# Changing the expert in four steps over two iterations, with two row buffers, earlier gathers and a second first-layer bank

## The chip, the cores and the metric

The kernel runs on one core of a Trainium2 chip. The core has TensorE (PE, matmuls into PSUM banks; PEld is its weight load), VectorE (DVE), ScalarE (ACT), GpSimd (POOL) and SyncE (SP), each with its own instruction stream; they wait for one another through semaphores. The metric is the device time of one execution in microseconds; lower is better.

## What is computed

Three stages follow one another. `_attn_ref` is attention with four sink keys and a window of 128 over 4 batches, 8 heads, 768 positions. `_moe_ref` is a dense layer, 512 to 2048 and back, with `h - tanh(h)` between. The third stage sends each of the 3072 tokens to one of eight experts:

```python
logits = x @ w_gate + modality_bias[modality_id]
e_idx = np.argmax(logits, axis=1)
...
for e in range(E):
    mask = e_idx == e
    if not mask.any():
        continue
    h = np.maximum(x[mask] @ w1[e], 0.0)
    out[mask] = gate_w[mask, None] * (h @ w2[e])
```

`w1[e]` is 512 x 1024 and `w2[e]` is 1024 x 512. In the profiled data the trace shows the weights of two experts loaded, so the expert changes once.

## The kernel before

**Front.** The dense layer works on eight chunks of 384 tokens. Chunk m has 16 column blocks f. `mlp_in` computes the first layer of block f into the bank `h_ps` (12 matmuls); ACT takes the tanh (L718), DVE subtracts it (L727, "the gate of f"), ACT and DVE split the result into a high and a low 16-bit half (`g_hi` L737, `g_lo` L747), and `mlp_out` multiplies them with `w_out` (9 matmuls). PE runs `mlp_in` of f+1 ahead of `mlp_out` of f. Since there is one bank, `mlp_in` of f+2 waits until the gate of f+1 has read it. In the last chunk the first expert is prepared between: DVE and ACT look for the largest weights (`look_over`), and split the eight weight pieces into `ew_hi` and `ew_lo` (L1474, L1478). Then the routing of the last chunk is computed.

**Expert stage.** Tokens are sorted by expert in a table `slots`, and worked off in blocks of 128, numbered j from 0 to 24. For a block, POOL loads its part of the table (`load_slots`, tile `slot_g`) and gathers its rows of `x2` (`gather`, tile `xg`); DVE finds the scale and ACT applies it (`scale_x`, L1723 to L1730); PE transposes (`transpose_x`, L1743, into `x_out`); ACT and DVE split (`xg_hi` L1749, `xg_lo` L1752). `hidden_products` is 96 small matmuls (L1766) in two halves c of four column groups; `relu` splits each half (`hid_hi` L1780, `hid_lo` L1783). `output_products` is 24 matmuls of 512 columns (L1817). `load_slots_again` fetches the gate weights (`slot_y`, L1791), DVE makes `y_scale` of them (`output_scale`, L1805), ACT scales the output (`y`, L1833), POOL scatters it (L1838).

Blocks 0 to 2 are "early" blocks of the first expert, and their code is written out. Block 3 is the joining block: `output_products` of block 2 alone, then `transpose_x` of 3, then `hidden_products` of 3 alone. From j = 4 a loop runs: in iteration j PE interleaves `hidden_products` of j with `output_products` of j-1, one large matmul with four small ones, and transposes j+1 after the 15th large one. At its start PE waits for `y_set` of at least j-1, which is `output_scale` of the iteration before, the last thing that DVE does in an iteration. The order on ACT and DVE is what `iteration` writes.

**Tables.** DVE computes the plan on one partition: `plan`, `plan_blocks` (raises `planned`), and `plan_late` (raises `planned_late`; every engine waits for it ahead of the loop, and SP ahead of loading the next expert). The loop's conditions, whether a block begins an expert, are read from this plan by `read` (L1609) and tested by a branch.

**Change of expert.** `load_turn` loads the eight pieces of the next expert as soon as the present one has been split. `look_ahead` runs in the iteration after the first block of an expert. `next_turn` runs in the last iteration of the old expert (13 begins the new one, so j = 12): new scales, then, when all hidden products of block 12 are done, the four pieces of `w1`; in the next iteration, when the outputs of block 12 are done, the four pieces of `w2`.

Of the kernel before, what the change touches and what calls it, by code (L numbers as in the profile page):

```python
# [25 lines left out]
P = 128  # L26
# [26 lines left out]
PIECES = 8  # L53
NEG = -1.0e9
# [63 lines left out]
def front(nc, dram, shared, attention):  # L118

    with ExitStack() as ctx:  # L120
# [59 lines left out]
        h_ps, x_out = h_bank[:, 0:CT], x_bank[:, 0:CT]  # L180
# [509 lines left out]
        def mlp_in(E, eng, m, f, between=None):  # L690
# [4 lines left out]
            if E == "pe":  # L695
# [4 lines left out]
                need(eng, q["g_done"], n)  # L700
                i = 0
                for x, r in ((1, xt_hi), (0, xt_lo), (0, xt_hi)):
                    if i == 2 * KD and between:
                        between()
                    for k in range(KD):
                        mm = eng.matmul(h_ps, w16[0][:, f, x * DM + k * P:x * DM + (k + 1) * P], r[:, par, k, :],  # L706
                                        start=(i == 0), stop=(i == 3 * KD - 1))
                        i += 1
                mm.then_inc(q["h_done"], 1)
            if E == "act":  # L710
# [7 lines left out]
                eng.activation(g_raw[:, f % 2, :], h_ps, ACT.Tanh, scale=batch_scale[:, b, 0:1]).then_inc(q["tanh_done"], 1)  # L718

        def mlp_gate(E, eng, m, f):  # L720
# [184 lines left out]
        def prepare_expert(E, eng, k):  # L905
# [9 lines left out]
            if k in (15, 17, 19, 21):  # L915
                shared.split(E, eng, 0, (k - 15, k - 14))
# [76 lines left out]
        def join(E, eng):  # L993
# [9 lines left out]
            if E == "dve":  # L1003
# [332 lines left out]
class Shared:  # L1336
# [33 lines left out]
    def over_attention(self, sb):  # L1370
# [73 lines left out]
    def set_scales(self, E, eng, s, bank=None):  # L1444
# [9 lines left out]
        need(eng, self.w_hi, PIECES * s)  # L1454
# [12 lines left out]
    def split(self, E, eng, s, pieces):  # L1467

        for i in pieces:
            scale = self.w_scale[:, 0:1] if i < KD else self.w_scale[:, 1:2]  # L1470
            hi, lo = self.hi[:, i, :], self.lo[:, i, :]
            if E == "act":
                eng.wait_ge(self.scaled, s + 1)
                eng.activation(hi, self.raw[i][:], ACT.Copy, scale=scale).then_inc(self.w_hi, 1)  # L1474
            if E == "dve":
                eng.wait_ge(self.scaled, s + 1)
                eng.wait_ge(self.w_hi, PIECES * s + i + 1)
                eng.scalar_tensor_tensor(lo, self.raw[i][:], scale, hi, ALU.mult, ALU.subtract).then_inc(self.w_lo, 1)  # L1478
# [74 lines left out]
    def plan_late(self, eng):  # L1553
# [11 lines left out]
        step(tt(metaf[:, 2, :], vec["first"][:], b[:], ALU.mult))  # L1565
# [9 lines left out]
def expert_stage(sb, sem, dram, shared, xt_ps, hid_ps, y_ps):  # L1575
# [10 lines left out]
    slot_g = sb("slot_g", [P, 2], I32)  # L1586
# [44 lines left out]
    def next_turn(E, eng, j):  # L1631
# [61 lines left out]
    def load_slots(E, eng, j):  # L1693

        if E == "pool":
# [341 lines left out]
```

## Time and profile before

| | |
|---|---|
| median of 3 runs | 1139.35 us (1139.07 to 1141.08) |
| profiled execution | 1141.86 us, span 1140.2 us |
| PE busy | 1017.1 us, 89% of the span |
| DVE, ACT, POOL busy | 729.6, 618.5, 397.3 us |
| mean granted clock of TensorE | 0.972 of full speed |

The span is from the first to the last instruction; what lies around it is 1.7 us. PE is the engine with the most work, so idle time of PE, and time in which its clock is half, is what an edit can take away or add.

### The profile page before, as it was taken

The page shows a single profiled execution, that of the slowest core. Times are in us where ns is not written, and L with a number is a line of the kernel's source. Part 1 is how long each engine was busy: PE and PEld are TensorE (multiplying, and loading weights), DVE is VectorE, ACT ScalarE, POOL GpSimd, SP SyncE. Part 2 cuts the span into 40 slices and gives each one's busy share as a digit, 9 for nine tenths or more (in the row PEclk, how much of TensorE's full clock was granted, in tenths as well). Part 3 has the DMA queues.
Part 4 walks back from the last instruction along what each step waited for, and adds up shares of the span by engine and source line. Part 5 has one row for each costly group of instructions (what it writes and reads, how often), then busy time and mean ns, then how long its engine had stood idle before and what let it go on. Part 6 is the DMA issues. An engine that isn't in the chain of part 4 may idle for free.

```text
span 1140.2 us, 24342 instructions
## 1 busy us (share of the span) xinstructions
PE 1017.1 (89%) x7840; PEld 664.2 (58%) x7840; DVE 729.6 (64%) x2388; ACT 618.5 (54%) x1421; POOL 397.3 (35%) x457
## 2 busy tenths in 40 slices
PE   1657888999999999999999999998896999789997
PEld 0534555565665665566566566654664677567774
DVE  6787978677977867887867876547563333443331
ACT  2675877575766766667666667445322222332221
POOL 3786876222345312325412321110122222122222
PEclk9976999999999999999999999999998999889999
DMA  9832111231212322311231130050023111001111
GB/s 284 282 97 53 34 34 34 75 109 34 61 37 63 62 90 58 69 35 34 38 90 34 34 61 2 1 203 2 29 79 136 43 46 56 28 23 52 46 46 45
DMA packets 24427, 75.14 MB, mean 66 GB/s; under 512 B 9680, under 2 KB 9808, under 8 KB 22800
## 3 DMA queue, kind: packets, MB, share of 16 engines
q1 hardware_dynamic: 15440, 60.58, 19.9%
q0 software_dynamic: 5728, 13.43, 3.8%
q8 instruction: 44, 0.72, 0.3%
q14 instruction: 47, 0.39, 0.1%
q10 hardware_dynamic: 3168, 0.02, 0.1%
HBM read 60.16 MB, written 14.12 MB: 65 GB/s over the span
## 4 chain that ended last, share of the span: by engine, by line
PE 67%; DVE 15%; ACT 6%; issue 6%; POOL 2%; DMA 2%; DVEq 0%; ACTq 0%; SPq 0%; POOLq 0%
PE h_ps L706 16%; PE acc L762 14%; PE pt_ps L1766 11%; PE h_ps L1817 6%; PE acc L1817 5%; PE x_out L665 4%; PE s_ps L542 2%; PE pt_ps L611 2%; DVE g_raw L727 2%; DVE qk_top L385 2%; DVE qk_exp L394 1%; PE s_ps L811 1%; DVE ew_lo L1478 1%; DVE g_lo L747 1%; ACT probs L557 1%
## 5 line engine op out<-in xcount | busy, mean ns | idle before, releaser
L762 PE MATMUL acc<-w_out_all,g_hi 128*128 128x512 f16 x768 | 228.3, 379 | 0.0
L706 PE MATMUL h_ps<-xt_hi,w_in_all 128*128 128x384 f16 x1024 | 211.1, 329 | 16.9 <-DVE g_raw L727 16.8
L762 PE MATMUL acc<-w_out_all,g_lo 128*128 128x512 f16 x384 | 145.4, 379 | 2.5 <-POOL w_out_all L350 1.2
L594 ACT ACTIVATE pt_hi<-pt_ps 128x256 f16<-128x256 f32 (+2 forms) x224 | 83.6, 380 | 110.0 <-PE pt_ps L611 106.0
L706 PEld LDWEIGHTS h_ps<-xt_hi,w_in_all 128*128 128x128 f16 x1024 | 97.6, 99 | 78.2 <-DVE g_raw L727 16.3
L98 POOL TENSOR_TENSOR tick<-tick 1x1 f32<-1x1 f32 x83 | 15.3, 184 | 313.0 <-ACT y L1833 97.8
L747 DVE SCALAR_TENSOR_TENSOR g_lo<-g_raw,batch_scale,g_hi 128x384 f16<-128x384 f32 x128 | 95.2, 743 | 33.1 <-ACT g_hi L737 30.7
L762 PEld LDWEIGHTS acc<-w_out_all,g_hi 128*128 128x128 f16 x768 | 75.0, 98 | 69.2
L598 DVE TENSOR_TENSOR pt_lo<-pt_ps,pt_hi 128x256 f16<-128x256 f32 (+2 forms) x224 | 94.3, 423 | 29.9 <-ACT pt_hi L594 28.2
L718 ACT ACTIVATE g_raw<-h_ps,batch_scale 128x384 f32<-128x384 f32 x128 | 74.3, 580 | 71.8 <-PE h_ps L706 70.5
L432 POOL TENSOR_TENSOR q_stack<-qk_raw,q_stack 64x768 f16<-64x768 f32 x31 | 50.8, 1639 | 165.5 <-ACT q_stack L428 165.5
L706 PE MATMUL h_ps<-xt_lo,w_in_all 128*128 128x384 f16 x512 | 106.1, 331 | 0.0
L575 ACT ACTIVATE normed<-probs,row_sum 128x260 f32<-128x260 f32 (+1 forms) x192 | 92.9, 484 | 21.1 <-DVE row_sum L570 20.9
L727 DVE SCALAR_TENSOR_TENSOR g_raw<-h_ps,batch_scale,g_raw 128x384 f32<-128x384 f32 x128 | 78.4, 612 | 37.9 <-ACT g_raw L718 36.5
L737 ACT ACTIVATE g_hi<-g_raw,batch_scale 128x384 f16<-128x384 f32 x128 | 78.0, 609 | 45.2 <-DVE g_raw L727 44.7
L1783 DVE SCALAR_TENSOR_TENSOR hid_lo<-pt_ps,hid_hi 128x512 f16<-128x512 f32 x50 | 34.6, 691 | 96.5 <-ACT hid_hi L1780 91.9
L557 ACT ACTIVATE probs<-probs,neg_max 128x260 f32<-128x260 f32 (+1 forms) x192 | 92.8, 483 | 5.8 <-DVE neg_max L552 5.7
L432 POOL TENSOR_TENSOR kl_stack<-qk_raw,kh_stack 128x1048 f16<-128x1048 f32 (+1 forms) x31 | 60.2, 1941 | 99.1 <-ACT kh_stack L428 98.4
L611 PE MATMUL pt_ps<-ident,normed 128*128 128x128 f32 x352 | 74.0, 286 | 22.7 <-ACT normed L575 22.6
L552 DVE CUSTOM_DVE_ANT_0 probs<-s_ps,mask 128x260 f32<-128x260 f32 (+1 forms) x180 | 73.1, 406 | 24.1 <-issue 22.9
L1766 PE MATMUL pt_ps<-xg_lo,ew_hi 128*128 128x128 f16 x800 | 79.0, 222 | 1.5 <-DVE xg_lo L1752 1.4
L409 POOL TENSOR_SCALAR qk_raw<-qk_raw,qk_scale 128x768 f32<-128x768 f32 (+2 forms) x62 | 61.0, 996 | 52.3 <-DVE qk_scale L400 52.3
(293 smaller groups left out, 2237.3 us busy)
## 6 DMA issues: line engine op xcount, KB each, us to landing
qk_raw<-in_qk SPq DMA_DIRECT2D x64, 454.0 KB, 6.1
raw<-in_w SPq DMA_DIRECT2D x16, 512.0 KB, 7.7
v_raw<-in_v SPq DMA_DIRECT2D x4, 1536.0 KB, 9.7
x_tokens<-x SPq DMA_DIRECT2D x24, 256.0 KB, 5.3
w_in_all<-in_w_in SPq DMA_DIRECT2D x4, 1024.0 KB, 13.2
w_out_all<-in_w_out SPq DMA_DIRECT2D x4, 1024.0 KB, 12.3
x_tokens<-g_raw SPq DMA_DIRECT2D x1, 1024.0 KB, 14.0
slots<-payload,dest POOLq DMA_INDIRECT x24
```

The lines of the kernel that those rows point to most:

```text
L432: eng.tensor_tensor(lo, raw[half], hi[half], ALU.subtract).then_inc(q["conv_lo"], 1)
L557: eng.activation(probs[:, r, cols], probs[:, r, cols], ACT.Exp, bias=neg_max[:, r:r + 1], scale=-1.0, accum_out=row_sum[:, r:r + 1]).then_ ...
L575: eng.activation(normed[:, u % 6, cols], probs[:, r, cols], ACT.Copy, scale=row_sum[:, r:r + 1])\
L594: eng.activation(pt_hi[:, at, :], out, ACT.Copy).then_inc(q["pt_hi_done"], 1)
L598: eng.tensor_tensor(pt_lo[:, at, :], out, pt_hi[:, at, :], ALU.subtract).then_inc(q["pt_lo_done"], 1)
L611: mm = eng.transpose(out[:, b, :], normed[:, u % 6, b * KB:b * KB + P], ident[:])
L706: mm = eng.matmul(h_ps, w16[0][:, f, x * DM + k * P:x * DM + (k + 1) * P], r[:, par, k, :], start=(i == 0), stop=(i == 3 * KD - 1))
L727: eng.scalar_tensor_tensor(g, h_ps, batch_scale[:, b, 0:1], g, ALU.mult, ALU.subtract).then_inc(q["g_done"], 1)
L747: eng.scalar_tensor_tensor(g_lo[f % 2][:], g, batch_scale[:, b, 1:2], g_hi[f % 2][:], ALU.mult, ALU.subtract)\
L762: mm = eng.matmul(acc[t][:, :], l[f % 2][:, t * P:(t + 1) * P], w16[1][:, f, x * DM:(x + 1) * DM], start=(f == 0 and i == 0), stop=(f == N ...
L1766: mm = eng.matmul(hid_ps[c][:, (f - 4 * c) * P:(f - 4 * c + 1) * P], w[:, k, f * P:(f + 1) * P], x[p][:, k * P:(k + 1) * P], start=(i == 0 ...
L1817: mm = eng.matmul(y_ps[bank][:, :], l[:, f * P:(f + 1) * P], rhs, start=(f == 0 and i == 0), stop=(f == KF - 1 and i == 2))
```

## The change

1. **Four steps.** The weights of the next expert are split in quarters: `w1` first half of the columns in iteration J-1 (J is the first block of the new expert) after half c = 0 of J-1 is done; `w1` second half at the head of iteration J; `w2` first two pieces in iteration J after `y_half`; `w2` last two at the head of iteration J+1. The head is ahead of `relu` of j-1. New scales are made by DVE in iteration J-1 ahead of `relu` of j. `look_ahead` moves from the iteration after the expert's first block to two iterations ahead of J (iteration J-2), and stands ahead of `relu` of j. `load_slots_again` moves ahead of the transposed rows. In an iteration without any step, ACT and DVE now test more conditions.
2. **Two row buffers.** `xg` and `slot_g` have two halves, so `gather` of j+2 waits for the transposes of j, not of j+1. The slots and rows of block 4 are fetched directly after those of block 3, ahead of the early scatters.
3. **Order.** `transpose_x` in an iteration comes after the 18th large matmul, not the 15th. In the joining block it stands inside the products, and the early `scale_x` goes ahead of the output of block 1. `plan_late`, with five more steps, moves from ahead of the joining block to behind it. SP loads the next expert after three gathers.
4. **Two banks.** In the last chunk `mlp_in` writes odd f into `pt_bank[1]`, and waits for one gate less.

```diff
+        def h_of(m, f):
+            return (pt_bank[1] if m == NC - 1 and f % 2 else h_bank)[:, 0:CT]
...
-                need(eng, q["g_done"], n)
+                need(eng, q["g_done"], n - 1 if m == NC - 1 and f else n)
...
                 stage_e.relu(E, eng, 2, 0)
-                shared.plan_late(eng)
...
-                stage_e.load_slots(E, eng, EARLY)
-                stage_e.gather(E, eng, EARLY)
+                stage_e.load_slots(E, eng, EARLY, EARLY % 2)
+                stage_e.gather(E, eng, EARLY, EARLY % 2)
+                eng.wait_ge(shared.planned, 1)
+                stage_e.load_slots(E, eng, EARLY + 1, 1 - EARLY % 2)
+                stage_e.gather(E, eng, EARLY + 1, 1 - EARLY % 2)
...
-        step(tt(metaf[:, 2, :], vec["first"][:], b[:], ALU.mult))
+        first, now, sel, short = vec["first"], metaf[:, 1, :], vec["n"], vec["t"]
+        w = MB - KD
+        step(ts(metaf[:, 2, :], b[:], 0.0, None, ALU.mult))
+        step(tt(sel[:, 0:w], now[:, 0:w], now[:, 2:w + 2], ALU.is_equal))
+        step(tt(sel[:, 0:w], sel[:, 0:w], first[:, 3:w + 3], ALU.mult))
+        step(tt(short[:, 0:w], first[:, 0:w], first[:, 2:w + 2], ALU.mult))
+        step(tt(sel[:, 0:w], sel[:, 0:w], short[:, 0:w], ALU.add))
+        step(tt(metaf[:, 2, 0:w], sel[:, 0:w], b[:, 0:w], ALU.mult))
...
+    def next_turn_begins(E, eng, j):
 
         if E in ("act", "dve"):
             s = read(eng, 4, j + 1, NE)
             with eng.If(s > 0):
-                shared.set_scales(E, eng, s)
-                eng.wait_ge(q["hid_mm"], 2 * j + 2)
-                shared.split(E, eng, s, range(KD))
+                eng.wait_ge(q["hid_mm"], 2 * j + 1)
+                shared.split_w1(E, eng, s, 0)
             s = read(eng, 4, j, NE)
             with eng.If(s > 0):
-                eng.wait_ge(q["y_mm"], j)
-                shared.split(E, eng, s, range(KD, PIECES))
+                eng.wait_ge(q["y_half"], j)
+                shared.split_w2(E, eng, s, 0)
+
+    def next_turn_ends(E, eng, j):
+
+        if E in ("act", "dve"):
+            s = read(eng, 4, j, NE)
+            with eng.If(s > 0):
+                eng.wait_ge(q["hid_mm"], 2 * j)
+                shared.split_w1(E, eng, s, 1)
+            s = read(eng, 4, j - 1, NE)
+            with eng.If(s > 0):
+                eng.wait_ge(q["y_mm"], j - 1)
+                shared.split_w2(E, eng, s, 1)
...
         if E == "dve":
+            next_turn_ends(E, eng, j)
             relu(E, eng, j - 1, 1)
             output_part(E, eng, j - 1, 1 - p, turn_of(eng, j - 1))
             scale_x(E, eng, j + 1, 1 - p)
+            look_ahead(E, eng, j)
+            next_scales(E, eng, j)
             relu(E, eng, j, 0)
+            next_turn_begins(E, eng, j)
             transpose_x(E, eng, j + 1, 1 - p)
-            look_ahead(E, eng, j)
-            next_turn(E, eng, j)
             output_scale(E, eng, j - 1, j - EARLY)
```

On POOL, where the early blocks end, the rows of before are these (tick is the one-element operation that carries the waits):

```order
L1702 DMA slot_g<-slots 128x2
L98 TENSOR_TENSOR tick<-tick 1x1 [waits e_slot_in]
L1710 DMA xg<-x_tokens,slot_g 128x512
L98 TENSOR_TENSOR tick<-tick 1x1 [waits e_y_out]
L1838 DMA out<-y,slot_e 3072x512
L98 TENSOR_TENSOR tick<-tick 1x1 [waits e_carried_3,e_y_out]
L1838 DMA out<-y,slot_e 3072x512
```

And these at the same place of the change:

```order
L1747 DMA slot_g<-slots 128x2
L99 TENSOR_TENSOR tick<-tick 1x1 [waits e_slot_in]
L1755 DMA xg<-x_tokens,slot_g 128x512
L1636 TENSOR_LOAD meta [waits planned]
L1636 ISA x2
L99 TENSOR_TENSOR tick<-tick 1x1 [waits e_carried_1]
L1747 ISA
L1747 DMA slot_g<-slots 128x2
L99 TENSOR_TENSOR tick<-tick 1x1 [waits e_carried_2,e_slot_in]
L1755 DMA xg<-x_tokens,slot_g 128x512
L99 TENSOR_TENSOR tick<-tick 1x1 [waits e_y_out]
L1884 DMA out<-y,slot_e 3072x512
```

The second fetch has moved ahead of the scatter of block 0. On DVE, at the end of the joining block, before:

```order
L1752 TENSOR_TENSOR xg_lo<-x_out,xg_hi 128x512 [waits e_xt_hi]
L1609 TENSOR_LOAD meta [waits planned]
L1609 ISA x2
L1965 UNCONDITIONAL_BRANCH [waits planned_late]
```

And in the change, where the plan's steps are left out in the middle:

```order
L1798 TENSOR_TENSOR xg_lo<-x_out,xg_hi 128x512 [waits e_xt_hi]
L1582 TENSOR_SCALAR vec_b<-metaf 1x44
L1583 TENSOR_SCALAR vec_t<-vec_b,pt_turn_end 1x44 [waits plan_late_step]
...
L1598 COPY metaf<-pt_turn_end 1x1 [waits plan_late_step]
L1599 CAST meta_late<-metaf 1x132 [waits plan_late_step]
L1636 TENSOR_LOAD meta [waits planned]
L1636 ISA x2
L2015 UNCONDITIONAL_BRANCH [waits planned_late]
```

The late plan, 18 rows in all, now stands between the last split of the joining block and the entry of the loop.

## Rows read from the trace of the kernel before

**Rows 1.** Waits of PE, 822 us to the end: total us, times, longest:
```profile
PE h_ps L1817 <- DVE y_scale L1805: 11.6, 2, 6.7
PE x_out L1743 <- ACT xg L1730: 6.9, 1, 6.9
PE acc L1817 <- DVE y_scale L1805: 6.1, 1, 6.1
```

**Rows 2.** Waits of PE, 740 to 822 us (the last chunk):
```profile
PE h_ps L706 <- DVE g_raw L727: 3.6, 3, 1.7
```

**Rows 3.** Timeline, last chunk, ACT: start, us, engine, line, operation [idle before]:
```profile
809.62 0.58 ACT L718 ACTIVATE g_raw<-h_ps,batch_scale 128x384 f32<-128x384 f32 x1 [0.34 <-PE h_ps L706]
```

**Rows 4.** Windows of iterations 4, 5, 10 to 14: length, busy PE, PEld, DVE, ACT, POOL, clock, DMA, GB/s:
```profile
868.70:886.38 17.68, 12.80 (x124) 8.97 (x125) 9.13 (x17) 6.81 (x13) 2.96 (x5) 0.89 0.11 31
886.38:898.86 12.48, 12.44 (x124) 9.04 (x124) 3.69 (x10) 3.07 (x6) 3.17 (x6) 0.89 0.26 55
942.82:953.80 10.98, 10.98 (x128) 8.20 (x125) 3.69 (x10) 3.09 (x6) 3.16 (x6) 1.00 0.15 47
953.80:964.83 11.03, 11.03 (x128) 8.20 (x125) 3.69 (x10) 3.14 (x6) 3.16 (x6) 1.00 0.16 48
964.83:982.75 17.92, 11.18 (x127) 8.19 (x125) 10.05 (x22) 7.46 (x10) 3.16 (x6) 0.96 0.10 30
982.75:1002.61 19.86, 13.71 (x125) 9.83 (x125) 8.48 (x14) 7.36 (x10) 3.16 (x6) 0.84 0.08 27
1002.61:1016.44 13.83, 13.83 (x124) 10.00 (x124) 3.70 (x10) 3.06 (x6) 3.16 (x6) 0.79 0.09 21
```

**Rows 5.** Timelines of the joining block, POOL, ACT, DVE, PE:
```profile
837.72 0.58 POOL L1702 DMA_DIRECT2D slot_g<-slots  x1 [0.45 <-issue]
...
841.80 1.03 POOL L1838 DMA_INDIRECT out<-y,slot_e  x1 [0.16 <-POOL tick L98]
...
847.09 0.69 ACT L1833 ACTIVATE y<-acc,ye_scale 128x512 f32<-128x512 f32 x1 [4.45 <-PE acc L1817]
...
843.28 0.16 DVE L1562 TENSOR_SCALAR vec_b<-metaf 1x44 f32<-1x44 f32 x1
...
846.71 0.22 DVE L1572 CAST meta_late<-metaf 1x132 int32<-1x132 f32 x1
...
868.70 0.60 PE L1817 MATMUL acc<-ew_hi,hid_lo 128*128 128x512 f16 x1 [0.82 <-issue]
```

**Rows 6.** DMA issues, 925 to 1100 us: queue, kind, count, KB, us to landing:
```profile
slot_y<-slots ACTq DMA_DIRECT2D x14, 1.0 KB, 1.7
out<-y,slot_y POOLq DMA_INDIRECT x14, 2.8
```

**Rows 7.** DMA issues, 848 to 866 us (while the next expert loads):
```profile
slot_g<-slots POOLq DMA_DIRECT2D x2, 1.0 KB, 4.0
```

**Rows 8.** Timelines of iteration 9, which begins at 931.83 us, ACT and DVE:
```profile
931.82 0.69 ACT L1833 ACTIVATE y<-acc,y_scale 128x512 f32<-128x512 f32 x1 [3.27 <-PE acc L1817]
...
933.03 0.69 DVE L1783 SCALAR_TENSOR_TENSOR hid_lo<-pt_ps,hid_hi 128x512 f16<-128x512 f32 x1 [1.30 <-ACT hid_hi L1780]
...
935.45 0.15 DVE L1727 TENSOR_SCALAR x_undo<-x_exp 128x1 int32<-128x1 int32 x1
...
939.59 0.69 DVE L1752 TENSOR_TENSOR xg_lo<-x_out,xg_hi 128x512 f16<-128x512 f32 x1 [0.93 <-ACT xg_hi L1749]
942.45 0.16 DVE L1805 TENSOR_TENSOR y_scale<-slot_y,y_part 128x1 f32<-128x1 f32 x1 [2.17 <-DMA slot_y<-slots]
```

**Rows 9.** The chain in order of time, a read and branch on DVE, and the next:
```profile
972.70 0.31 DVEq L1609
...
973.64 0.31 DVEq L1609
```

**Rows 10.** Timelines of iterations 4 and 12, DVE: the work of the change of expert:
```profile
879.09 4.60 DVE L1415 TENSOR_REDUCE tops<-raw 128x1 f32<-128x1024 f32 x4 [0.24 <-issue]
...
977.67 4.87 DVE L1478 SCALAR_TENSOR_TENSOR ew_lo<-raw,ew_scale,ew_hi 128x1024 f16<-128x1024 f32 x4 [1.22 <-ACT ew_hi L1474]
```

More of the change, by code:

```diff
@@ L717, in mlp_in @@
                 need(eng, q["g_hi_done"], n - 1)
[L718 removed]
+                eng.activation(g_raw[:, f % 2, :], h_of(m, f), ACT.Tanh, scale=batch_scale[:, b, 0:1]).then_inc(q["tanh_done"], 1)
         def mlp_gate(E, eng, m, f):
@@ L915, in prepare_expert @@
             if k in (15, 17, 19, 21):
-                shared.split(E, eng, 0, (k - 15, k - 14))
+                shared.split_first(E, eng, (k - 15, k - 14))
             if k == 23:
@@ L1453, in set_scales @@
             source = bank[:, 0:2 * P].rearrange("p (i n) -> p i n", i=2)
-        need(eng, self.w_hi, PIECES * s)
+        need(eng, self.w_hi, PARTS * s)
         step = chain(eng, self.scale_step, 7 * s)
@@ L1465, in set_scales, with split_part, split_first, split_w1 @@
         eng.tensor_tensor(at, self.both[:, 0:1], self.both[:, 1:2], ALU.mult).then_inc(self.scaled, 1)
-    def split(self, E, eng, s, pieces):
-        for i in pieces:
[L1470 to L1478, printed above, removed]
+    def split_part(self, E, eng, s, n, i, cols, counted=1):
+        scale = self.w_scale[:, 0:1] if i < KD else self.w_scale[:, 1:2]
+        raw, hi, lo = self.raw[i][:, cols], self.hi[:, i, cols], self.lo[:, i, cols]
+        if E == "act":
+            eng.wait_ge(self.scaled, s + 1)
+            eng.activation(hi, raw, ACT.Copy, scale=scale).then_inc(self.w_hi, counted)
+        if E == "dve":
+            eng.wait_ge(self.scaled, s + 1)
+            eng.wait_ge(self.w_hi, PARTS * s + n + 1)
+            eng.scalar_tensor_tensor(lo, raw, scale, hi, ALU.mult, ALU.subtract).then_inc(self.w_lo, counted)
+    def split_first(self, E, eng, pieces):
+        for i in pieces:
+            self.split_part(E, eng, 0, KD + i, i, slice(0, FE), counted=KD + 1 if i == 0 else 1)
+    def split_w1(self, E, eng, s, half):
+        for i in range(KD):
+            self.split_part(E, eng, s, KD * half + i, i, slice(half * FE // 2, (half + 1) * FE // 2))
+    def split_w2(self, E, eng, s, pair):
+        for i in (2 * pair, 2 * pair + 1):
+            self.split_part(E, eng, s, 2 * KD + i, KD + i, slice(0, FE))
     def plan_iotas(self, eng):
@@ L1629, in look_ahead, with next_scales @@
                 shared.sum_rows(E, eng, s)
-    def next_turn(E, eng, j):
+    def next_scales(E, eng, j):
+        if E == "dve":
+            s = read(eng, 4, j + 1, NE)
+            with eng.If(s > 0):
+                shared.set_scales(E, eng, s)
+    def next_turn_begins(E, eng, j):
         if E in ("act", "dve"):
@@ L1699, in load_slots, with gather @@
                 row = read(eng, 0, j, NE * N - P)
-            need(eng, q["gathered"], 16 * (j - EARLY))
+            need(eng, q["gathered"], 16 * (j - EARLY - 1))
             carry_waits(eng, tick, 7, q["carried_1"], j - EARLY)
-            eng.dma_start(slot_g[:], dram["slots"][bass.ds(row, P), :]).then_inc(q["slot_in"], 16)
-    def gather(E, eng, j):
+            eng.dma_start(slot_g[:, p, :], dram["slots"][bass.ds(row, P), :]).then_inc(q["slot_in"], 16)
+    def gather(E, eng, j, p):
         if E == "pool":
             eng.wait_ge(q["slot_in"], 16 * (j - EARLY + 1))
-            if not (isinstance(j, int) and j == EARLY):
-                eng.wait_ge(q["xt_done"], j)
+            if not (isinstance(j, int) and j < EARLY + 2):
+                eng.wait_ge(q["xt_done"], j - 1)
             carry_waits(eng, tick, 2, q["carried_2"], j - EARLY)
-            eng.indirect_dma_start(out=xg[:], out_offset=None, in_=dram["x2"],
-                                   in_offset=bass.IndirectOffsetOnAxis(ap=slot_g[:, 0:1], axis=0)).then_inc(q["gathered"], 16)
+            eng.indirect_dma_start(out=xg[:, p, :], out_offset=None, in_=dram["x2"],
+                                   in_offset=bass.IndirectOffsetOnAxis(ap=slot_g[:, p, 0:1], axis=0)).then_inc(q["gathered"], 16)
     def scale_x(E, eng, j, p):
         n = j - EARLY
+        x = xg[:, p, :]
         if E == "dve":
@@ L1871, in iteration @@
             scale_x(E, eng, j + 1, 1 - p)
+            look_ahead(E, eng, j)
+            next_scales(E, eng, j)
             relu(E, eng, j, 0)
+            next_turn_begins(E, eng, j)
             transpose_x(E, eng, j + 1, 1 - p)
-            look_ahead(E, eng, j)
-            next_turn(E, eng, j)
             output_scale(E, eng, j - 1, j - EARLY)
         if E == "pool":
-            load_slots(E, eng, j + 2)
-            gather(E, eng, j + 2)
+            load_slots(E, eng, j + 2, p)
+            gather(E, eng, j + 2, p)
             output(E, eng, j - 1, 1 - p)
```

62 lines of the change are left out of this document (33 added, 29 removed).

## The prediction

> **What bounds the kernel now.** I read the waits of PE first. From 822 us to the end PE waited 11.6 and 6.1 us for `y_scale` and 6.9 us for the scaled rows `xg` [rows 1]: 24.6 us, all at the joining block, in iteration 4 and at the change of expert. In the last chunk it waited 3.6 us for the gate [rows 2]. Then the windows that run from one start of an iteration to the next [rows 4]. An undisturbed iteration takes 10.98 us with PE busy throughout, so such iterations can't get shorter. Iteration 4 took 17.68, 5 took 12.48, 11 took 11.03, 12 to 14 took 17.92, 19.86 and 13.83. The clock column shows the second cost: a wait of PE is followed by a stretch at the lower of its two levels (mean 0.89 in iteration 5, 0.79 in iteration 14, where PE never idled and still lost 2.85 us). So there are 24.6 us of waits and some 6 us of clock to be had (17.68, 12.48, 17.92, 19.86 and 13.83 hold 26.9 us above five times 10.98, and the joining block the rest); the rest of PE's work is not touched.
>
> **Last chunk.** The second bank lets `mlp_in` run before the gate of the block ahead, but `mlp_out` still needs that block's `g_lo`, and the gates come one behind the other on DVE, which is also splitting the first expert. DVE has the same list as before, so PE's 3.6 us [rows 2] mostly move to the wait for `g_lo`. What is won is what ACT then waits less for its last tanh: it sat idle 0.34 us before it [rows 3]. I take 0.4; the bounds are 0 and 3.6.
>
> **Joining block.** All times here are on the clock of the old trace.
> - POOL: the scatter of block 0 was issued at 841.80, one slot load (837.72) and one gather behind [rows 5]. A second pair, 4.08 us by those two rows, plus a read of some 0.5 us, is now ahead of it: 846.4. It lands 2.8 us later [rows 6]: 849.2.
> - ACT's output of block 1 needs that landing, and stood at 847.09 [rows 5]: now 849.2. Behind it on ACT is `relu` of block 2, half 1; from output to the end of `hid_lo` takes 1.9 us (931.82 to 933.72, [rows 8]): 851.1.
> - PE starts the lone output products at 847.1, does 12 of 24 and the transposes of block 3 (12 x 0.22 + 0.44: these and 96 x 0.055 make up 10.98 [rows 4]): 850.2. It waits 0.9 us, does the other 12 (853.8), and hidden products with the transposes of 4 (5.3 + 0.44): 859.6. The wait of 6.9 us for `xg` [rows 1] is gone, because the rows of block 4 were fetched seven us earlier.
> - But `plan_late` is now behind DVE's last split of block 4. PE transposes block 4 at 857.8; the split ends some 1.9 us later, 859.7. The plan took 3.65 us (843.28 to 846.93 [rows 5]), and five more steps of 0.22 us make 4.75: 864.4. Every engine waits for it before the loop. The way into the loop was 0.82 us [rows 5], of which the read is now done before; I take 0.5. PE's loop begins at 864.9, less 0.4 from the chunk: 864.5 instead of 868.70. **Won: 4.2**, and there is a new wait of PE of 5.3 us for the plan. Bounds: 2.5 (the scatter lands 1.7 us later) and 9 (no wait for the plan).
>
> **Iteration 4.** `look_ahead` leaves it: four reductions of 4.60 us on DVE [rows 10], behind which `y_scale` stood. The 17.68 us fall to 10.98 plus the slow clock after the new wait, 1.5 us as in iteration 5 (12.48), so 12.5. But SP now loads the 4 MB of the next expert during it, since it waits for the plan and three gathers. The slot load that `y_scale` needs takes 1.7 us alone [rows 6]; POOL's small load under such traffic took a median 4.0 [rows 7]. I add 0.6: 13.1. **Won: 4.6** (bounds 3 and 6). Iteration 5 then has no wait ahead of it, 12.48 to 10.98: **won 1.5**.
>
> **Ordinary iterations.** Each has more reads with a branch: ACT 6 for 4, DVE 7 for 4. One costs 0.94 us on DVE [rows 9]; on ACT, where no two stand bare, I take 0.85. They count only where the engine is waited for. With T the start on PE: ACT's output at T, two tests, `hid_hi` at T+1.75, `hid_lo` at T+2.35 (before T+1.2); from there to `x_undo` 2.42 us (933.03 to 935.45 [rows 8]): T+4.8; ACT's scaling and one test, `hid_hi` of c = 0 at T+5.8; slot load and two tests, T+8.7; PE's transposes after the 18th product are ready at T+8.5; `xg_hi` 8.7, `xg_lo` 9.35, `y_scale` 10.1. PE needs it at about T+10.7. Before, it was ready at T+10.6 [rows 8], since three tests stood between `xg_lo` and it (939.59 to 942.45). So 0.6 us is spare: cost nothing, with 0.4 us once, in iteration 20, where the outer loop turns. Bounds: 0 and 1.5 us for each of 16 iterations.
>
> The Trainium skill (Runtime: NRT & Kernel Launch, Instruction fetch mechanics) says that a taken branch to a target outside the pages already held has to wait for a fetch. The rows show 0.94 us for a test whose branch is taken over its body, with nothing larger, so the sum goes by the row; by the rule the longer bodies could make some tests dearer, which is the slower rival below.
>
> **Change of expert, iterations 11 to 14.** Each is worked out as a chain on ACT and DVE.
> - 11: `look_ahead` begins on DVE at T+5.75 and takes 4.6; with the row sums and the test for new scales, `hid_lo` of c = 0 starts at 11.65; two tests, `xg_lo` 13.6, `y_scale` 14.3. **14.6 us.**
> - 12: the outer loop turns (0.8 on ACT); new scales, 1.9 us, are done at 9.4; `hid_lo` 9.5; four half-size splits (half of 4.87 [rows 10]) from 10.5 to 13.0; `xg_lo`, `y_scale` 13.7. **14.0.**
> - 13: four half-size splits at the head, so `hid_lo` of half 1 at 4.05 to 4.7, just ahead of PE's need at 5.25; `x_undo` 6.45, two tests, `hid_lo` 8.4; two tests; two full splits behind ACT's, 11.4 to 13.8; `xg_lo`, `y_scale` 14.5. **14.8.**
> - 14: two full splits at the head, `hid_lo` 5.2 to 5.9 (PE waits 0.65); the rest as in an ordinary iteration, 1.5 to 2 us later: **13.2.**
>
> Sum 56.6 against 11.03 + 17.92 + 19.86 + 13.83 = 62.64 [rows 4]: **won 6.0**. PE idles between 2 and 4 us ahead of 12, 13 and 14. Whether its clock falls there matters little, as DVE sets the end of these iterations. Bounds: 0 won (each chain 1.5 us longer) and 18.7 (all four at 10.98).
>
> **Sum.** 4.2 + 4.6 + 1.5 + 6.0 - 0.4 = 15.9 us. The profiled execution took 1141.86 us (span 1140.2 and 1.7 around it) and would take 1126.0; it stands 2.5 us above the median of the runs. From the median: 1139.35 - 15.9 = **1123.5**.
>
> **The rivals.**
> - *The steps hide almost wholly.* For it: the sequencers run ahead of queued work whose waits are met, so the tests may cost less than 0.9 us. Against it: most instructions here do wait. Iterations 11 to 14 at 12 us each win 14.6 instead of 6.0, and with the small terms at their better bounds: about 1112.
> - *The late plan and the late load take the gain.* The plan behind the joining block is at its dear bound, and the 4 MB delay the slots and rows of blocks 6 and 7, so that iteration 4 wins 3; with 4 from the change of expert: 2.5 + 3 + 1.5 + 4 - 0.4 = 10.6, so 1129.
> - *Only the join is gained; the four steps cost what they save.* Iterations 11 to 14 stay at 62.6: 1129.5. For it: DVE's list is as long as before.
> - *Slower: the tests become the bound.* Each of the 16 ordinary iterations (5 to 10 and 15 to 24) ends when ACT and DVE are through their tests. With 0.6 us spare, six tests in series would have to cost 0.27 us more apiece to add 1.0 us to an iteration; 15.9 / 16 = 1.0 us each is where it decides, and at 1.3 us each the time is 1144. Against it: the price of a test is read from a row.
> - *No change:* nothing in the trace speaks for it; the waits for `xg` and `look_ahead` are surely gone.
>
> **How the numbers follow.** Forecast 0.55 (its own range 1118 to 1127), steps hidden 0.15, late load 0.12, steps cost what they save 0.10, slower 0.06, within 0.2% 0.02 (2.3 us, about what a measurement of this kernel can tell from no change). The range from 1114 to 1131 leaves out part of the first rival and the last two, about 2 in 10. Faster 0.92, same 0.02, slower 0.06.
>
> **What would show it.** PE waits some 5 us before the first matmul of the loop, released by the plan; no wait for `xg`. The next expert's load begins near 866 us, after the loop's start. Iteration 4 takes about 13 us, ordinary ones 10.98. Iterations 11 to 14 take 13 to 15 us each, with `y_scale` as PE's releaser. If ordinary iterations exceed 11.2 us, the price of the tests was wrong; if 11 to 14 are near 11, the chains; if the loop begins before 862, the plan was not in the way.

## The result and the profile after

The changed kernel takes 1127.51 us (median of 4 runs, 1126.34 to 1129.42), beside 1140.21 us for the kernel before (1139.07 to 1143.89). The ratio is 0.9885 (95% interval 0.9857 to 0.9912): 1.15% faster. The forecast of 1123.5 us was 4.0 us too low. The stated range of 1114 to 1131 held; the forecast's own narrower one, 1118 to 1127, was missed by 0.5 us. The profiled execution took 1126.34 us, span 1124.7 us, 15.5 us less than before.

The waits of PE from 822 us to the end, beside [rows 1]:

```profile
PE acc L1863 <- DVE y_scale L1851: 6.6, 2, 3.9
PE acc L1863 <- issue: 5.8, 1, 5.8
PE h_ps L1863 <- DVE y_scale L1851: 4.6, 3, 3.0
PE h_ps L1863 <- DVE hid_lo L1829: 2.2, 2, 1.6
PE h_ps L1863 <- issue: 1.7, 1, 1.7
```

The wait for `xg` is gone, and a wait "issue" of 5.8 us is new: it is the wait ahead of the loop. What PE waits for `y_scale` fell from 17.7 to 11.2 us. The two waits for `hid_lo` are 0.64 us, which was there before too, and 1.61 us in the joining block. In the last chunk, beside [rows 2], the three waits for the gate are gone, and there are these:

```profile
PE s_ps L866 <- DVE payload L851: 3.2, 1, 3.2
PE acc L766 <- DVE g_lo L751: 1.3, 1, 1.3
```

The iterations 4, 5, 10, 11, 12, 13, 14 and 15, one line each, in windows with the columns of [rows 4]:

```profile
863.65:878.52 14.87, 13.64 (x125) 9.77 (x125) 3.69 (x10) 2.55 (x5) 1.95 (x4) 0.83 0.82 299
878.52:889.50 10.98, 10.98 (x124) 8.17 (x125) 3.60 (x10) 3.17 (x6) 3.15 (x6) 1.00 0.16 54
933.46:944.44 10.98, 10.98 (x128) 8.18 (x126) 3.60 (x10) 3.20 (x6) 3.16 (x6) 1.00 0.15 48
944.44:958.30 13.86, 11.16 (x128) 8.19 (x126) 8.42 (x16) 7.27 (x14) 3.15 (x6) 1.00 0.14 38
958.30:972.41 14.11, 11.15 (x124) 8.18 (x125) 7.79 (x22) 5.64 (x10) 3.15 (x6) 1.00 0.24 47
972.41:987.60 15.19, 11.33 (x125) 8.15 (x125) 8.73 (x16) 7.71 (x12) 3.37 (x6) 1.00 0.11 35
987.60:1000.80 13.20, 12.80 (x124) 9.21 (x125) 5.90 (x12) 5.26 (x8) 3.27 (x6) 0.87 0.09 22
1000.80:1011.78 10.98, 10.97 (x124) 8.19 (x125) 3.60 (x10) 3.18 (x6) 3.15 (x6) 1.00 0.15 48
```

Iterations 11 to 14 last 56.36 us together against 62.64, with the DVE work of the change (8.42, 7.79, 8.73, 5.90 us busy) spread over four of them where it lay in two and in iteration 4. Iteration 4 lasts 14.87 us against 17.68.

**Where the 15.5 us came from.** In the profiled executions of all kernels here the first 810 us differ by up to 3.9 us, also between kernels that are alike there. So I count from one instruction near the end of the last chunk: the last group of PE's transposes of `xe` there, which begins with its 1.0 us wait for `xg_lo`. Before and after it reads:

```profile
812.97 0.63 PE L1743 MATMUL x_out<-ident,xe 128*128 128x128 f32 x4 [1.01 <-DVE xg_lo L1752]
```

```profile
810.35 0.63 PE L1789 MATMUL x_out<-ident,xe 128*128 128x128 f32 x4 [1.01 <-DVE xg_lo L1798]
```

Up to there the changed kernel is 2.62 us ahead: 3.15 us of that were gained before the last chunk began, and the chunk itself is 0.53 us longer (each from the DVE row that writes `x` at the end of one chunk to the same row of the next, 740.63 to 812.96 against 743.78 to 815.58). From the mark to the loop's first matmul it was 55.73 us and is 53.30 (won 2.43). Then come iteration 4 (2.81), 5 to 10 (1.50) and 11 to 14 (6.28); the rest lost 0.14. Sum 2.62 + 2.43 + 2.81 + 1.50 + 6.28 - 0.14 = 15.5. Without the 3.15 us ahead of the last chunk, where the two kernels are alike, 12.35 us are left: the change's own share. Below, "the rest from the mark" is the span less the start of this instruction: 327.23 us before, 314.35 after.

### The profile page after: what moved, and what is told of

Same layout as the page of the kernel before. It is cut to its first block, busy times and chain, and to the rows that moved or that the text cites. A ratio compares the mean times of both kernels' runs of the same rounds, so it can differ in the third digit from the quotient of the medians.

```text
span 1124.7 us, 24805 instructions
## 1 busy us (share of the span) xinstructions
PE 1010.4 (90%) x7840; PEld 660.9 (59%) x7840; DVE 728.9 (65%) x2397; ACT 620.1 (55%) x1425; POOL 396.8 (35%) x457
## 4 chain that ended last, share of the span: by engine, by line
PE 63%; DVE 16%; issue 7%; ACT 6%; POOL 3%; DMA 2%; ACTq 1%; DVEq 1%; POOLq 0%; SPq 0%
PE h_ps L710 16%; PE acc L766 15%; PE pt_ps L1812 9%; PE x_out L669 5%; PE h_ps L1863 4%; PE acc L1863 4%; PE s_ps L546 2%; PE pt_ps L615 2%; DVE qk_top L389 2%; DVE qk_exp L398 1%; PE s_ps L815 1%; DVE g_raw L731 1%; DVE ew_lo L1483 1%; DVE pt_lo L602 1%; ACT probs L561 1%
## 5 line engine op out<-in xcount | busy, mean ns | idle before, releaser
L710 PE MATMUL h_ps<-xt_hi,w_in_all 128*128 128x384 f16 x960 | 197.1, 328 | 13.2 <-DVE g_raw L731 13.2
L710 PEld LDWEIGHTS h_ps<-xt_hi,w_in_all 128*128 128x128 f16 x960 | 91.6, 98 | 67.5 <-issue 10.1
L722 ACT ACTIVATE g_raw<-h_ps,batch_scale 128x384 f32<-128x384 f32 x120 | 69.5, 579 | 64.7 <-PE h_ps L710 63.1
L710 PE MATMUL h_ps<-xt_lo,w_in_all 128*128 128x384 f16 x480 | 99.0, 329 | 0.0
L731 DVE SCALAR_TENSOR_TENSOR g_raw<-h_ps,batch_scale,g_raw 128x384 f32<-128x384 f32 x120 | 73.5, 612 | 31.8 <-ACT g_raw L722 30.7
L1812 PE MATMUL pt_ps<-xg_hi,ew_lo 128*128 128x128 f16 x800 | 78.3, 221 | 0.0
```

Source lines behind the costliest of these rows:

```text
L710: mm = eng.matmul(h_of(m, f), w16[0][:, f, x * DM + k * P:x * DM + (k + 1) * P], r[:, par, k, :], start=(i == 0), stop=(i == 3 * KD - 1))
L731: eng.scalar_tensor_tensor(g, h_of(m, f), batch_scale[:, b, 0:1], g, ALU.mult, ALU.subtract).then_inc(q["g_done"], 1)
L1812: mm = eng.matmul(hid_ps[c][:, (f - 4 * c) * P:(f - 4 * c + 1) * P], w[:, k, f * P:(f + 1) * P], x[p][:, k * P:(k + 1) * P], start=(i == 0 ...
```

## The experiments

Each edit is against the changed kernel unless it says otherwise.

**The change once more** (`after_again`), no edit.

> The change itself once more. If the 1.6 us wait of PE in the joining block and the slot load of 3.2 us ahead of it were of that one execution, they are absent here, the loop begins about 49 us after the last chunk's last matmul, and the span is some 1.6 us shorter than 1124.7; if they belong to the change, both are there again.

1125.56 us (1125.42 to 1127.74), ratio 0.9883 (0.985 to 0.9917). The rest from the mark (812.29, span 1123.8) is 311.51 us, 2.84 less than in the first profile. The loop begins at 863.79, 51.50 after the mark and not 53.30, and the 1.6 us wait for `hid_lo` isn't there. POOL's timeline shows why, first of the first execution, then of this one (a `tick` that waits marks the landing of the slots):

```profile
835.38 0.58 POOL L1747 DMA_DIRECT2D slot_g<-slots  x1 [0.45 <-issue]
838.61 0.18 POOL L99 TENSOR_TENSOR tick<-tick 1x1 f32<-1x1 f32 x1 [2.64 <-DMA slot_g<-slots]
...
844.42 1.03 POOL L1884 DMA_INDIRECT out<-y,slot_e  x1 [0.16 <-POOL tick L99]
```

```profile
836.54 0.58 POOL L1747 DMA_DIRECT2D slot_g<-slots  x1 [0.39 <-issue]
838.64 0.18 POOL L99 TENSOR_TENSOR tick<-tick 1x1 f32<-1x1 f32 x1 [1.52 <-DMA slot_g<-slots]
```

The same 1 KB load took 3.2 us once and 2.1 us here. It had also been issued later in the first execution, 25.03 us after the mark against 24.25, because the writing of `slots` ahead of it had landed 0.8 us later. Both shifted everything behind them on POOL, the scatter of block 0 among it, by 2.1 us; the loop's start moved by 1.8.

Iteration 4 was 13.77 us here and 14.87 there, and that is mostly the clock. The wait ahead of the loop was the same, 5.8 us, but behind it six matmuls of 512 columns took 0.60 to 0.64 us in the first execution and four here, so PE was busy 13.64 us against 12.83. The window here, beside the first of those above:

```profile
863.79:877.56 13.77, 12.83 (x124) 9.30 (x125) 3.69 (x10) 2.55 (x5) 1.95 (x4) 0.87 0.88 321
```

The load of `slot_y` was issued 0.8 us later for it; from issue to `y_scale` it took 5.77 us against 5.48. So of the 2.84 us between two executions of one kernel, some 1.8 are two small DMAs ahead of the loop, 0.8 are the clock behind one and the same wait, and 0.3 a third DMA. Why these differ isn't shown.

**One bank** (`one_bank`):

```diff
-            return (pt_bank[1] if m == NC - 1 and f % 2 else h_bank)[:, 0:CT]
+            return h_bank[:, 0:CT]
...
-                need(eng, q["g_done"], n - 1 if m == NC - 1 and f else n)
+                need(eng, q["g_done"], n)
```

> The changed kernel with the second first-layer bank taken out again; all else is kept. Theory A (the second bank only gathers three short waits of PE into one of 3.2 us at the ranking matmul, behind which the clock falls): the last chunk, from the store of the chunk before to the end of its own products, gets 0.5 to 1.4 us shorter than with two banks, the three waits of 1.7, 1.4 and 1.0 us come back, and no matmul of the second layer takes 0.6 us. Time 1126 to 1127.5. Rival B (the second bank wins what PE waited for the gate): the chunk gets 1 to 3 us longer, time 1129 to 1131.

**The second bank alone, in the kernel before** (`bank_only`, the same lines put in there):

> The kernel before with nothing but the second first-layer bank in the last chunk. Theory A (waits are gathered, not removed): the last chunk is between 0.3 us shorter and 1.0 us longer, the time is that of before within 1 us. Rival B (PE's 3.6 us of waits for the gate are won): 1136 to 1138.

Without the bank: 1124.93 us (1123.85 to 1125.31), ratio 0.987 (0.9842 to 0.9898); the chunk is 0.5 us shorter (71.82 us, 72.33 with two banks, 71.80 before). The bank alone: 1140.15 us, ratio 0.9998 (0.998 to 1.0016), chunk 72.34 us. The chunk is counted between the two DVE rows that write `x`. Both pairs of kernels put the bank's price at 0.5 us, below what the total time can tell: `one_bank` is 0.6 us faster than `after_again`, 2.6 us faster than the first measurement of the change. PE's timeline with two banks shows it:

```profile
797.49 0.18 PE L866 MATMUL s_ps<-chosen,tri 128*128 128x24 bf16 x1 [3.16 <-DVE payload L851]
...
798.77 0.63 PE L766 MATMUL acc<-w_out_all,g_lo 128*128 128x512 f16 x1
```

And with one:

```profile
799.07 0.17 PE L866 MATMUL s_ps<-chosen,tri 128*128 128x24 bf16 x1 [0.95 <-DVE payload L851]
...
799.76 0.38 PE L766 MATMUL acc<-w_out_all,g_lo 128*128 128x512 f16 x1
```

With one bank PE waits 1.71, 1.38 and 0.48 us for the gate and 0.95 us for the ranking's `payload`, 4.5 us in all, and the clock stays up: the matmul of 512 columns takes 0.38 us. With two banks it waits 1.28 us for `g_lo` and 3.16 us for `payload`, 4.4 us in all, and behind the second wait the same matmul takes 0.63 us. The windows of 3.6 us at that place, with two banks and with one:

```profile
797.40:801.00 3.60, 3.51 (x12) 1.38 (x13) 2.16 (x7) 0.61 (x1) 0.00 (x0) 0.56 0.03 7
```

```profile
797.70:801.30 3.60, 2.65 (x16) 1.04 (x15) 2.45 (x10) 0.82 (x2) 0.00 (x0) 1.00 0.01 2
```

The granted clock is 0.56 with two banks, most of it at the lower level, and 1.00 with one. All nine profiles with two banks have this wait of 3.2 us and a clock of 0.55 to 0.66 behind it; the four with one bank have 1.00. So the bank saved 0.1 us of waits, since `payload` came only 0.3 us earlier after the start of the chunk, and slow matmuls made PE's busy time in the chunk 0.7 us longer (66.88 us for 66.19).

**The late plan in DVE's idle time** (`plan_mid`):

```diff
             scale_x(E, eng, j, p)
+            shared.plan_late(eng)
             relu(E, eng, j - 1, 1)
...
             transpose_x(E, eng, j + 1, 1 - p)
-            shared.plan_late(eng)
```

> The changed kernel with the late plan on DVE moved from behind the joining block to between the scaling of block 3 and relu of block 2, where DVE sat idle 4.6 us. Theory A (the late plan alone holds the loop's start): the wait of 5.8 us ahead of the loop falls below 1 us, iteration 4 loses no clock (another 1 to 1.5 us), time 1120.5 to 1122. Rival B (the loop's entry, the gather of block 5 or the load of the next expert, which then starts earlier and meets that gather, holds it): the wait stays above 3 us or comes back in iteration 4, time 1125 or more.

1120.52 us (1119.22 to 1122.57), ratio 0.9838 (0.9809 to 0.9867). In the changed kernel DVE's timeline ends the joining block so, with 16 further steps of the plan between, and PE's goes on:

```profile
857.19 0.69 DVE L1798 TENSOR_TENSOR xg_lo<-x_out,xg_hi 128x512 f16<-128x512 f32 x1 [1.09 <-ACT xg_hi L1795]
857.79 0.17 DVE L1582 TENSOR_SCALAR vec_b<-metaf 1x44 f32<-1x44 f32 x1
...
862.32 0.22 DVE L1599 CAST meta_late<-metaf 1x132 int32<-1x132 f32 x1
```

```profile
857.47 0.39 PE L1812 MATMUL pt_ps<-xg_hi,ew_hi 128*128 128x128 f16 x4
863.65 0.60 PE L1863 MATMUL acc<-ew_hi,hid_lo 128*128 128x512 f16 x1 [5.79 <-issue]
```

In the experiment the plan runs from 843.73 to 848.54, while DVE would have waited more than 4 us for ACT. The wait ahead of the loop shrinks from 5.79 to 0.79 us, and the loop begins 46.51 us after the mark instead of 51.50. The rest from the mark is 305.52 us: 5.99 less than in `after_again`, of which 5.0 are the wait and the rest is iteration 4 (12.8 us for 13.8), whose granted clock is 1.00 now. It is still 1.8 us above an ordinary one, 1.6 of them idle time of PE.

**The scatter of block 0 ahead of the second fetch** (`scatter_first`):

```diff
+                stage_e.early_iteration(E, eng, 1, 1)
                 eng.wait_ge(shared.planned, 1)
                 stage_e.load_slots(E, eng, EARLY + 1, 1 - EARLY % 2)
                 stage_e.gather(E, eng, EARLY + 1, 1 - EARLY % 2)
-                stage_e.early_iteration(E, eng, 1, 1)
```

> The changed kernel with the scatter of block 0 put back ahead of the second pair of slot load and gather on POOL. Theory A (the second pair delays the scatter, the scatter delays the output of block 1 on ACT, and with it relu of block 2): PE's wait of 1.6 us in the joining block goes, block 4's rows still come in time, and the loop starts 1.0 to 1.6 us earlier; time 1126 to 1127. Rival B (the rows of block 4 come late in its place): PE waits for xg, no gain.

1125.26 us (1124.57 to 1132.29), ratio 0.989 (0.9854 to 0.9927). The rest from the mark is 312.06 us, against 311.51 in `after_again`: no gain. ACT's output of block 1 came 0.6 us earlier than with the change's order (845.00, 34.16 after the mark, against 845.93, 34.79 after it, in `one_bank`), but PE waits for it in neither. The wait of 1.6 us that I had blamed on this order came with the two late small DMAs of that one execution. With the scatter first, ACT's output waits for PE alone; with the change's order it waits for the scatter, at no cost in the end.

**One test more on ACT and DVE** (`extra_test`):

```diff
     def next_turn_ends(E, eng, j):
 
         if E in ("act", "dve"):
+            s = read(eng, 4, j, NE)
+            with eng.If(s > NE - 1):
+                eng.nop()
```

> The changed kernel with one more read and branch, never taken into its body, at the head of every iteration on ACT and DVE. Theory A (the tests stand in the chain that ends an iteration, with 0.0 us spare in even and 0.8 us in odd iterations): even ones grow by about 0.85 us, odd ones by 0 to 0.2, so 7 to 8 us over 16 ordinary iterations, and 2 to 3 us over iterations 11 to 14; time 1136 to 1139. Rival B (tests hide behind the matmuls): ordinary iterations stay at 10.98 us, time 1128 to 1130.

1133.78 us (1131.17 to 1137.56), ratio 0.9948 (0.9931 to 0.9965): slower than the change, and between what the two theories had. Two ordinary iterations take 22.50 us (11.38 and 11.12) instead of 21.96, with waits of 0.2 to 0.3 us for `y_scale`, and iterations 11 to 14 take 59.1 instead of 56.4 us. So the ordinary iterations of the changed kernel have next to nothing to spare: one test more, some 0.8 us of ACT's and DVE's time, adds 0.27 us to each of them on average. That is some 4.3 us over the 16 ordinary iterations, where theory A had 7 to 8, so part of the test was hidden; where isn't shown. ACT's timeline of the changed kernel shows the alternation (iteration 10):

```profile
933.46 0.69 ACT L1879 ACTIVATE y<-h_ps,y_scale 128x512 f32<-128x512 f32 x1 [1.71 <-PE h_ps L1863]
935.65 0.60 ACT L1826 ACTIVATE hid_hi<-pt_ps 128x512 f16<-128x512 f32 x1 [1.51 <-issue]
```

Two tests stand between: 2.19 us from start to start here, 1.59 us in iteration 9. DVE makes `y_scale` at 944.13 and PE goes on at 944.44; in iteration 9 it made it at 932.39 for 933.46. Where PE does wait, it starts 0.14 us after the end of `y_scale` (878.22 and 0.16 long, for 878.52); by that iteration 9 had 0.8 us to spare and iteration 10 nothing.

**The order of before inside the iterations** (`steps_undone`), with the transposes left after the 18th product, and then **the same with the transposes after the 15th** (`undone_14`). ACT's list, shortened; DVE's likewise. `next_turn` is that of before, and `look_ahead` stays in iteration J-2:

```diff
-            next_turn_ends(E, eng, j)
             relu(E, eng, j - 1, 1)
             scale_x(E, eng, j + 1, 1 - p)
-            look_ahead(E, eng, j)
             relu(E, eng, j, 0)
-            load_slots_again(E, eng, j - 1)
-            next_turn_begins(E, eng, j)
             transpose_x(E, eng, j + 1, 1 - p)
+            load_slots_again(E, eng, j - 1)
+            look_ahead(E, eng, j)
+            next_turn(E, eng, j)
```

> The changed kernel with the order of before in the iterations: all four pieces of w1 behind the hidden products, all four of w2 behind the outputs, look_ahead and the new scales at the end of the iteration; row buffers, gathers, plan and banks as changed. Theory A (the four steps win by overlap, about 10 us in iterations 11 to 15): iterations 12, 13 and 14 take 17.9, 19.9 and 13.8 us as before the change, iteration 11 some 16 us, time 1137 to 1139. Rival B (the steps cost what they save, and the gain at these iterations comes from moving look_ahead or from the earlier gathers): 12 and 13 take under 16 us, time below 1131.

> The order of before inside the iterations (as in steps_undone), and the transposes back behind the 15th large product; join, buffers, gathers and second bank as in the change. Theory A (the 25 us of steps_undone came from the 18th product standing behind three tests, the four steps are worth only the change of expert): ordinary iterations go back to 10.98 us with no wait for y_scale, iterations 11 to 14 take about 16, 18, 20 and 14 = 68 us against 56.4, so the time is some 11.5 us above the change: 1137 to 1140. Rival B (the tests and not the transposes make the ordinary iterations long): they stay above 11.5 us and the time above 1150.

`steps_undone`: 1164.95 us, ratio 1.0223 (1.0193 to 1.0253), 25 us slower than before, which no theory of mine had. `undone_14`: 1140.34 us, ratio 1.0002 (0.9981 to 1.0023). Two ordinary iterations of the first and the change of expert of the second:

```profile
918.01:930.32 12.31, 11.15 (x124) 8.19 (x125) 3.69 (x10) 3.17 (x6) 3.15 (x6) 1.00 0.14 43
930.32:942.51 12.19, 11.15 (x125) 8.19 (x125) 3.69 (x10) 3.09 (x6) 3.15 (x6) 1.00 0.13 43
```

```profile
945.14:961.03 15.89, 11.28 (x127) 8.19 (x125) 8.65 (x17) 7.39 (x14) 3.15 (x6) 0.95 0.11 33
961.03:981.62 20.59, 13.64 (x124) 9.80 (x125) 10.66 (x26) 8.21 (x14) 3.15 (x6) 0.83 0.16 32
981.62:1001.35 19.73, 13.58 (x124) 9.75 (x125) 8.48 (x14) 7.35 (x10) 3.15 (x6) 0.85 0.08 27
1001.35:1015.19 13.84, 13.84 (x125) 10.00 (x125) 3.69 (x10) 3.18 (x6) 3.15 (x6) 0.79 0.09 21
```

With the transposes back, ordinary iterations take 10.98 us again, so the 1.2 to 1.3 us too many came from the transposed rows: three products later, with the slot load and three tests still behind them. The later place of the transposes is thus free only together with the moved tests and slot load. The change of expert takes 70.05 us in `undone_14`, 7.4 us more than before: 4.9 in iteration 11, where `look_ahead` now sits, and 2.7 in iteration 12, whose cause isn't shown. Moving `look_ahead` out of iteration 4 therefore gains nothing by itself: it is paid again at the change. It is the new order on ACT and DVE, with the four steps in it, that makes the difference: `transposes_14`, the next run, differs from `undone_14` in nothing else and takes 56.5 us for 70.05. How much of it is the splitting in steps, and how much the new places of `look_ahead`, of the scales and of the slot load, no run separates.

**Transposes after the 15th product, nothing else** (`transposes_14`):

```diff
-            if i == 17:
+            if i == 14:
```

> The change with the transposes back behind the 15th large product, nothing else. Theory A: ACT and DVE reach the transposed rows only at about T+8.7 in either case, so ordinary iterations stay at 10.98 us and the time within 0.2% of the change (1125.5 to 1129.5). Rival B: the scaled rows are not yet there after the 15th product when the steps stand ahead of them; PE then waits up to 1 us in iterations 12 to 14, and the time is 1 to 3 us above the change.

1127.41 us (1125.19 to 1127.8), ratio 0.9887 (0.9853 to 0.992); the rest from the mark is 312.91 us, 1.4 more than in `after_again`. PE now waits 0.25 and 1.02 us for `xg` in iterations 12 and 14. Both theories were partly right: the total hardly differs, and the waits are there. Most of the 1.4 us is elsewhere: every second ordinary iteration takes 11.1 us in place of 10.98.

**All three mends together** (`combined`: `one_bank`, `plan_mid`, `scatter_first`), and **with SP's wait for three gathers taken out as well** (`combined_early_load`):

```diff
-        eng.wait_ge(q["gathered"], 16 * 3)
         with eng.Fori(1, NE)
```

> The changed kernel with one bank, the late plan in DVE's idle stretch and the scatter of block 0 ahead of the second pair, all three at once. Theory A: the gains add up to 7 to 9 us, time 1118.5 to 1121. Rival B: they share one wait, time 1122 or more.

> The combined kernel, with the wait of SP for three gathers taken away, so that the next expert loads from about 850 us on. Theory A (in iteration 4 PE waits 1.2 us because the slot load that y_scale needs takes 5.7 us beside the 4 MB load): that load is over before iteration 4 needs its slots; but the rows of block 5 are gathered beside it and land near 862 us. Net between 1 us faster than combined and 1 us slower. Rival B (the gather beside the load is on the path, as at 856 us of the kernel before, where it took 8.4 us): 3 us or more slower than combined.

1119.6 us (1118.12 to 1122.1), ratio 0.9823 (0.98 to 0.9845), and 1116.54 us (1115.49 to 1119.02), ratio 0.9798 (0.9777 to 0.982). The rests from the mark are 305.60 and 304.11 us: the early load wins 1.5 us, where at most 1 us had been expected, and the remainder of the distance lies ahead of the mark. From the mark `combined` is no faster than `plan_mid` alone (305.52 us), so the plan is what it gains there; the bank's 0.5 us lie in the chunk. The waits of PE that are left in the last one from 822 us to the end:

```profile
PE acc L1863 <- DVE y_scale L1851: 6.6, 2, 3.9
PE h_ps L1863 <- issue: 1.7, 1, 1.7
PE h_ps L1863 <- DVE y_scale L1851: 1.3, 1, 1.3
PE acc L1863 <- issue: 0.8, 1, 0.8
PE h_ps L1863 <- DVE hid_lo L1829: 0.6, 1, 0.6
```

Iteration 4 takes 10.98 us there. The wait ahead of iteration 13 is 1.3 us and not 3.0 only because PE was slower: behind the same wait of 2.70 us ahead of iteration 12 the granted clock was 0.88 here and 1.00 in the changed kernel, and both iterations last 14.11 us. This version beats both kernels.

## Why the prediction was right, and by how much not

- **Sign and the main mechanisms: right; the size too high.** The forecast counts 15.9 us from 1139.35. The medians give 12.7 us, from 1140.21: 3.2 us of the 4.0 are terms that were too large, and the rest is the median of before, which came out 0.9 us higher with a fourth run. The wait for `xg` is gone, the late plan holds up the loop (5.3 us forecast, 5.79 measured), SP's load begins at 864.4 behind the loop's start, and `y_scale` is what PE waits for in iterations 11 to 14.
- **Joining block: right in size in one execution, too high in the other.** Forecast 3.8 us apart from the chunk. From the mark to the loop 55.73 us fell to 51.50 (4.2 us) in `after_again`, and only to 53.30 (2.4 us) in the first profile, where two small DMAs landed 0.8 and 1.1 us later. The step on the scatter, a PE wait of 0.9 us, was wrong: without these late DMAs PE doesn't wait there. Another was wrong the other way: the plan ended at 862.5 and PE started 1.1 us later, where I took 0.5 us for the way into the loop.
- **Last chunk: the sign was wrong.** Forecast +0.4 us, measured -0.5. The step "PE's 3.6 us mostly move to the wait for `g_lo`" was wrong: 1.3 us did, 2.2 us moved to the wait ahead of `s_ps`, and the clock was missed, for behind that one wait TensorE ran at its lower level.
- **Iteration 4: too high.** Forecast 4.6 us won; 2.8 in the first profile, 3.9 in `after_again`. Two terms were mis-sized. The slow clock was put at 1.5 us, after iteration 5 of before; PE's busy time above 10.98 us was 2.7 us in the first profile and 1.9 in `after_again`. The slot load beside the 4 MB was put at 0.6; PE's idle time in the iteration was 1.2 and 0.9. In the first profile that load took 5.7 us to landing (issued at 872.45, `y_scale` at 878.22), where it takes 1.7 alone [rows 6]. The Trainium skill (DMA: Bandwidth & Descriptors, Queues, rings and completion order) says that each DMA engine takes its queues in turn, a packet at a time. That fits, as the eight loads of weights fill the engines (DMA share 0.82 in the window of iteration 4), though no run here separates the queues. `combined` and `combined_early_load` show this term alone, since neither has slow matmuls there: iteration 4 is 12.7 us in the first, and 10.98 with the load begun before the loop.
- **Iterations 5 to 10: exact** (1.5 us). **Ordinary iterations: right that they cost nothing, wrong in what is spare.** I wrote 0.6 us; it is about 0.8 in one and nothing in the next. `extra_test` used that up. By the Trainium skill (Runtime: NRT & Kernel Launch, Instruction fetch mechanics), where a branch that leaves the pages held waits for a fetch, longer bodies could make some tests dearer; two tests on ACT do differ, 1.51 and some 0.9 us idle, by turns, but the runs don't show whether fetching is why.
- **Iterations 11 to 14: near in the sum** (6.0 forecast, 6.28 measured), chain by chain 14.6, 14.0, 14.8, 13.2 against 13.86, 14.11, 15.19, 13.20: iteration 11 was 0.7 us too high and 13 was 0.4 too low, so part of the closeness is luck. That DVE sets the end of these iterations held: in seven profiles of kernels with this order, 12 took 14.1 us whether the clock in it was 0.88 or 1.00. The wait of 0.65 us for `hid_lo` in 14 isn't there in the first profile, where PE ran at 0.87; in `transposes_14`, with the clock at 1.00, it is 0.96. What I had not seen is how much of this is `look_ahead`: the old order, with `look_ahead` moved to iteration 11, costs 70.05 us.
- **The rivals.** "The late plan and the late load take the gain" came true in half: it had 2.5 us for the join and 3 for iteration 4, and the first profile has 2.4 and 2.8. Its 1129 us is nearer to the median than the forecast is. What it had wrong is the change of expert, 4 us for 6.3, and in `after_again` the join gives 4.2. Nor was it the slots and rows of blocks 6 and 7 that cost iteration 4 its gain, but the clock and `slot_y`. "The steps hide almost wholly" fell with 56.4 us. "The tests become the bound" is one test away: `extra_test` is it, in small. "The steps cost what they save" fell with the 56.4 us too, and with `undone_14`.

The sum, 15.9 us, compares with 12.35 us in the first profile and with 15.2 in `after_again` (327.23 - 311.51, less the chunk's 0.5). By the medians the change is worth 12.7 us (first comparison) and 14.0 (second). What remains open is how often such small loads are slow, and how long the clock stays low behind one wait: two profiles can't say.

## What to carry to other kernels

Ask of work that moves out of an idle place where it will be done instead: the plan behind the joining block cost 5 us, and the same steps in a gap of DVE cost nothing. Several short waits of TensorE can be cheaper than one longer wait (4.5 us in four waits against 4.4 in two, and the chunk with the two was 0.5 us longer), so look at the durations of the matmuls behind a wait before counting it as saved. And take the time from a fixed instruction to the end when start-ups differ by more than the effect that is looked for.

## What was unexpected of the hardware

- Waits of 1.71, 1.38 and 0.95 us, 5.5 and 3.1 us apart, left the granted clock at 1.00; one of 3.16 us was followed by 3.6 us at 0.56, and 512-column matmuls of 0.63 us instead of 0.38.
- The length of the wait alone doesn't decide it. The wait of 2.70 us ahead of iteration 12 was followed by an iteration at 1.00 in `after`, `after_again`, `one_bank`, `scatter_first` and `combined`, and at 0.88 in `plan_mid` and `combined_early_load`. Behind 5.8 us ahead of the loop the matmuls were slow for some 5 us in `after` and 3.5 in `after_again`.
- The first slot load of 1 KB in the joining block took 2.1 to 2.2 us in the profiles of `after_again` and of all ten other experiments, 2.4 in the kernel before, and 3.2 us in one, of the same program as `after_again`; beside 4 MB of weights such a load, of `slot_y`, took 5.7.
- Two reads with a test on ACT took 1.5 us in one iteration and 0.9 in the next, in turn.
